# The place of six exponentials in ScalarE's queue: pairs 41 to 43 take the odd slot, pairs 44 to 46 the even one

## The chip, the cores and the metric

The kernel runs on one core of a Trainium2 chip. The metric is the device time in microseconds (us) of one execution; lower is better. The engines are TensorE (PE in the profile, its weight loads PEld), VectorE (DVE), ScalarE (ACT), GpSimd (POOL) and SyncE (SP, which only issues DMAs here). Each works through a queue of its own in the order in which the program wrote it, and waits on semaphores for the others.

## The reference

All in float32. First, attention for 4 batches of 8 heads, 576 tokens, head dimension 64: scores = q kᵀ / 8; of each row of scores only the 32 largest are kept, softmax over them, times v. Then two MLP blocks over the 4 x 576 tokens of width 512. The first mixes x by a real part of a two-dimensional Fourier transform, u = x + Re(FFT2(x)), normalises u over the width, and adds relu(un w1) w2 (512 to 2048 to 512). The second does the same without the transform and with a gain vector. The mask of the 32 largest is what VectorE spends its time on.

```python
kth = np.partition(scores, -top_k, axis=-1)[..., -top_k:-top_k + 1]
scores = np.where(scores >= kth, scores, -1000000000.0)
attn = np.exp(scores - np.max(scores, axis=-1, keepdims=True))
attn = attn / (np.sum(attn, axis=-1, keepdims=True) + 1e-09)
```

## The kernel before

**Tiles, pairs and slots.** The attention is cut into 144 tiles of 128 rows by 576 scores, 36 to a batch, two tiles to a pair (72 pairs). TensorE and ScalarE work in slots, one for each tile: slot s transposes the masked probabilities of tile s (`probs_T`, L684) and copies them out of PSUM (`probs_out`, L927). Each slot also carries pieces of the other work: one or two units of an MLP (`mlp1`, L735: 512 to 128 hidden columns; `mlp2`, L752: back to 512), in odd slots the product with v (`values`, L706 or L700) and its copies, and in slots 76 to 80 the ten pieces of the Fourier transform of batch 1 (`dft_piece`, L779 to L796; copied out by `piece_out`, L958). Which unit lies in which slot is a fixed plan; slots 82 and 87 hold two units. Before a group of units starts, its tokens are turned (`un_T`, L811 on TensorE in slots 86, 87 and 88; `un_out`, L976 and L980 on ScalarE).

**VectorE goes by pairs.** `pair(n)` finds the 32 largest of tiles 2n and 2n+1 in four rounds of MAX8 (L1140), with three rounds of MATCH_REPLACE8 (L1146) between them, and then masks: it multiplies the exponentials `ex` by (score >= 32nd largest) (L1153). The mask waits for the exponentials (`s_exp`); the transposes of slot s wait for the mask of tile s (`s_masked`). After pairs 40, 41 and 42 VectorE also combines the transform's pieces of batch 1 (`combined`, L1217 to L1236), and after pairs 61, 62 and 63 those of batch 2.

**Exponentials.** ScalarE writes `ex` for both tiles of a pair (`exps`, L920, behind a small scaling of the maxima, L915, that waits for the first round of MAX8 of both tiles). In most of the kernel it does so in the even slot s for the pair s/2 + 1, right behind `probs_out(s)`. Where `late_exps(s)` holds, it does so in the odd slot behind it, right behind `probs_out(s + 1)`:

```python
if s % 2 == 0 and s + 2 < TILES and s not in (...) and not late_exps(s):
    exps(s + 2)
    exps(s + 3)
if s % 2 == 1 and late_exps(s - 1):
    exps(s + 1)
    exps(s + 2)
```

Behind them in the same slot of ScalarE's queue come the two copies of the hidden unit (`relu_out`, L989 and L990), which TensorE's next unit and GpSimd's subtraction (L512) wait for, then `un_out`, `piece_out`, the copies of the product with v (L943, L951, L938), and the conversions of the weights for coming units (L1009, L1004). NT is 36. `late_exps` holds before the change for s // 2 in 43, 44, 45 and in 61, 62, 63, that is, for the exponentials of pairs 44, 45, 46 and of pairs 62, 63, 64.

**Scores.** From pair 36 on the scores come back from HBM, where they were set aside; ScalarE issues the load of pair s/2 + 2 in even slots (`scores_in`, L909).

Of the kernel before, what the change touches and what calls it, by code (L numbers as in the profile page):

```python
# [14 lines left out]
NT = NHP * TPP  # L15
# [102 lines left out]

def late_exps(s):

    return s // 2 in (NT + 7, NT + 8, NT + 9, 3 * NT // 2 + 7, 3 * NT // 2 + 8, 3 * NT // 2 + 9)


def scaled_by_act(p):
# [93 lines left out]
def build(nc, q, k, v, g2, w_raw, seq_t, wid_t, alt_t, w_low, sc_ahead, out):  # L218
# [4 lines left out]
    with ctx:  # L223
# [651 lines left out]
        def _(act):  # L875
# [163 lines left out]
            for s in range(SLOTS):  # L1039
                pieces = [(b, i) for b in range(B) for i in range(PIECES) if piece_slot(b, i) == s]  # L1040
                if s < TILES:
                    probs_out(s)
                    if s == START[0]:
                        for t in turns_at(s):
                            un_out(t)
                    if 0 <= s - 2 < AHEAD:
                        scores_aside(s - 2)
                    if s + RING < KEPT:
                        if s not in SCORED.values():
                            scores_out(s + RING)  # L1050
                    elif s % 2 == 0 and s + RING < TILES:
                        scores_in((s + RING) // 2)
                    if s % 2 == 0 and s < 2 * KF:
                        weights_high(s + 1)
                    if 0 <= s - 2 < AHEAD:
                        store_aside(s - 2)
                    if s % 2 == 0 and s + 2 < TILES and s not in (START[0] - 3, START[0] - 1, START[0] + 1) and not late_exps(s):
# [5 lines that stand above are left out]
# [324 lines left out]
```

## Time and profile before

| | |
|---|---|
| Time, median of 3 runs (lowest, highest) | 1359.7 us (1359.5, 1363.7) |
| The profiled execution's own time | 1362.1 us |
| Its span | 1360.3 us |
| Busy share of the span: PE, PEld, DVE, ACT, POOL | 92%, 75%, 81%, 59%, 26% |
| The chain that ended last: PE, DVE, all others | 57%, 36%, 7% |
| Mean granted clock of TensorE | 0.977 of full speed |

The profile is that of one execution. The span runs from the first to the last instruction; the time around it is 1.8 us. A busy share is a mean over stages with different limits. The chain is the work that ended last, followed back from the last instruction, at each step to what released it or to the instruction before it on its engine.

### The profile page before, as it was taken

How to read it: one execution, taken by the hardware profiler on the slowest of the kernel's cores; microseconds unless marked ns; L12 is line 12 of the kernel's file. 1: busy time of each engine (PE TensorE's matmuls, PEld its weight loads, DVE VectorE, ACT ScalarE, POOL GpSimd, SP SyncE). 2: the span in 40 equal slices, each digit the busy share in tenths (PEclk: the TensorE clock that was granted, in tenths of full speed). 3: DMA queues.
4: the chain of work that ended last, by engine and by line, in shares of the span. 5: the costliest groups of instructions: out<-in, count | busy, mean ns of one | idle time of the engine just before them, and what ended most of it. 6: DMA issues, size and time to landing. Idle time of an engine off the chain costs nothing.

```text
span 1360.3 us, 22775 instructions
## 1 busy us (share of the span) xinstructions
PE 1252.0 (92%) x7944; PEld 1024.3 (75%) x7944; DVE 1101.4 (81%) x2196; ACT 798.4 (59%) x1586; POOL 356.6 (26%) x327
## 2 busy tenths in 40 slices
PE   5776778999999899999988999999989999999999
PEld 3444444787777778788876888887679999999997
DVE  7999999899999989999999779975484454646453
ACT  4777765578777646776665557664353434343442
POOL 2444430122232431223335123333030111212110
PEclk9989978999999899999999999999999999999999
DMA  7899993567757757777885577753244343333342
GB/s 249 321 338 340 327 325 145 186 223 252 244 194 259 236 189 251 267 259 241 263 285 197 168 231 238 259 195 129 80 153 142 123 148 117 128 115 127 119 148 85
DMA packets 118259, 282.21 MB, mean 207 GB/s; under 512 B 29825, under 2 KB 29826, under 8 KB 118146
## 3 DMA queue, kind: packets, MB, share of 16 engines
q1 hardware_dynamic: 106386, 233.55, 51.7%
q10 hardware_dynamic: 10368, 42.47, 8.3%
q0 software_dynamic: 1392, 4.73, 1.1%
q8 instruction: 65, 1.06, 0.3%
q14 instruction: 48, 0.39, 0.1%
HBM read 237.44 MB, written 42.73 MB: 206 GB/s over the span
## 4 chain that ended last, share of the span: by engine, by line
PE 57%; DVE 36%; issue 5%; ACT 1%; POOL 1%; DMA 1%; SPq 0%; ACTq 0%; DVEq 0%
PE Big L752 23%; DVE top L1140 15%; PE Big L735 15%; DVE wk L1146 14%; PE Sp L735 7%; DVE ex L1153 3%; PE Tp L684 3%; PE Sp L779 2%; PE Tp L706 2%; PE Sp L791 1%; DVE st L1232 1%; PE Tp L811 1%; PE Big L779 1%; PE Sp L642 1%; PE Big L791 0%
## 5 line engine op out<-in xcount | busy, mean ns | idle before, releaser
L752 PE MATMUL Big<-wr,hh 128*128 128x512 f32 x1152 | 361.4, 395 | 0.0
L735 PE MATMUL Big<-uh,wr 128*128 128x256 f32 (+1 forms) x1400 | 320.9, 319 | 7.1 <-ACT hh L990 6.8
L1140 DVE MAX8 top<-wk 128x8 f32<-128x576 f32 x432 | 304.3, 745 | 0.0
L735 PEld LDWEIGHTS Big<-uh,wr 128*128 128x128 f32 x1400 | 236.5, 191 | 26.3 <-issue 16.5
L752 PEld LDWEIGHTS Big<-wr,hh 128*128 128x128 f32 x1152 | 217.6, 189 | 41.1
L752 PE MATMUL Big<-wr,hl 128*128 128x512 f32 x576 | 238.7, 414 | 4.8 <-DVE wr L1285 4.6
L512 POOL TENSOR_TENSOR hl<-hf,hh 128x256 fp32r<-128x256 f32 (+1 forms) x126 | 108.5, 861 | 452.5 <-ACT hh L990 452.5
L735 PE MATMUL Big<-ul,wr 128*128 128x256 f32 (+1 forms) x700 | 218.6, 312 | 0.0
L1146 DVE MATCH_REPLACE8 wk<-top,wk 128x576 f32<-128x576 f32 x288 | 211.4, 741 | 0.0
L684 PE MATMUL Tp<-ident,ex 128*128 128x128 f32 x720 | 117.1, 289 | 47.2 <-DVE ex L1153 38.3
L927 ACT ACTIVATE pT<-Tp 128x640 f32<-128x640 f32 x144 | 101.1, 702 | 88.1 <-PE Tp L684 87.9
L684 PEld LDWEIGHTS Tp<-ident,ex 128*128 128x128 f32 x720 | 86.5, 146 | 87.6 <-issue 50.8
L990 ACT ACTIVATE hh<-Big 128x384 fp32r<-128x384 f32 (+1 forms) x175 | 75.5, 432 | 118.1 <-PE Big L735 118.1
L1153 DVE SCALAR_TENSOR_TENSOR ex<-sc,top,ex 128x576 f32<-128x576 f32 x144 | 124.6, 902 | 18.8 <-ACT ex L920 18.7
L752 PEld LDWEIGHTS Big<-wr,hl 128*128 128x128 f32 x576 | 108.5, 188 | 34.8 <-issue 15.7
L735 PEld LDWEIGHTS Big<-ul,wr 128*128 128x128 f32 x700 | 133.5, 191 | 0.0
L1140 DVE MAX8 top<-sc 128x8 f32<-128x576 f32 x144 | 101.6, 746 | 16.6 <-ACT sc L886 9.5
L1146 DVE MATCH_REPLACE8 wk<-top,sc 128x576 f32<-128x576 f32 x144 | 105.7, 741 | 0.0
L920 ACT ACTIVATE ex<-sc,nmx 128x576 f32<-128x576 f32 x144 | 104.0, 769 | 2.3
L506 POOL TENSOR_TENSOR wr<-wf,wr 128x1024 fp32r<-128x1024 f32 x32 | 75.3, 2368 | 111.3 <-DVE top L1140 109.3
L989 ACT ACTIVATE hf<-Big 128x256 f32<-128x256 f32 (+1 forms) x126 | 52.2, 414 | 82.0 <-PE Big L735 82.0
L706 PE MATMUL Tp<-pT,vn 128*64 128x128 f32 x1280 | 87.9, 286 | 12.4 <-ACT pT L927 11.9
(136 smaller groups left out, 1832.1 us busy)
## 6 DMA issues: line engine op xcount, KB each, us to landing
wf<-in_weights SPq DMA_DIRECT2D x208, 512.0 KB, 3.6
wr<-w_low SPq DMA_DIRECT2D x252, 256.0 KB, 4.3
sc<-in_weights SPq DMA_DIRECT2D x48, 512.0 KB, 3.2
sc<-sc_ahead ACTq DMA_DIRECT2D x36, 576.0 KB, 5.6
w_low<-wr SPq DMA_DIRECT2D x32, 512.0 KB, 6.6
sc_ahead<-U ACTq DMA_DIRECT2D x18, 576.0 KB, 5.2
sc_ahead<-un ACTq DMA_DIRECT2D x9, 576.0 KB, 4.1
sc_ahead<-yb ACTq DMA_DIRECT2D x9, 576.0 KB, 6.5
```

The costliest lines, as they stand in the source:

```text
L506: pool.tensor_tensor(wr[:, r, :, 1, :], wf[:, j % WFS, :, :], wr[:, r, :, 0, :].bitcast(f32), ALU.subtract).then_inc(s_wlow, 1)
L512: pool.tensor_tensor(hl[:, n % 2, 0:w], hf[:, n % 2, 0:w], hh[:, n % 2, 0:w].bitcast(f32), ALU.subtract).then_inc(s_hl[0], 1)
L684: last = nc.tensor.transpose(Tp[:, c * P:(c + 1) * P], ex[:, s % RING, c * P:(c + 1) * P], ident[:, :])
L706: last = nc.tensor.matmul(OT[h * D:(h + 1) * D, :], vn[:, par, c, h, 0:D], pT[:, h, c * P:(c + 1) * P], start=(c == 0), stop=(c == C - 1))
L735: last = nc.tensor.matmul(hidden(n), a[:, kd * P:(kd + 1) * P], x[:, kd, 0:P * SIZE[p]], start=(kd == 0 and j == 0), stop=(kd == KD - 1 an ...
L752: last = nc.tensor.matmul(Ac[:, j, :], a[:, n % 2, j * P:(j + 1) * P], w, start=(f == 0 and m == 0), stop=(f == KF - 1 and m == 2))
L920: nc.scalar.activation(ex[:, s % RING, 0:S], sc[:, s % RING, :], ACT.Exp, bias=nmx[:, s % RING:s % RING + 1], scale=1.0 / np.sqrt(D)).then ...
L927: nc.scalar.activation(pT[:, s % 2, :], Tp[:, 0:C * P], ACT.Copy).then_inc(s_pT_sb, 1)
L990: nc.scalar.activation(hh[:, n % 2, 0:w], hidden(n), ACT.Relu).then_inc(s_h_sb, 1)
L1140: nc.vector.max(top[:, s % RING, r, :], src).then_inc(s_top, 1)
L1146: nc.vector.match_replace(out=wk[:, a, :], in_to_replace=top[:, s % RING, r, :], in_values=src, imm_value=STRUCK).then_inc(s_struck, 1)
L1153: nc.vector.scalar_tensor_tensor(out=ex[:, s % RING, 0:S], in0=sc[:, s % RING, :], scalar=top[:, s % RING, ROUNDS - 1, 7:8], in1=ex[:, s % ...
```

## The change

One line: the set for which `late_exps` holds. The first three of its six members move from 43, 44, 45 to 40, 41, 42.

```diff
 def late_exps(s):
 
-    return s // 2 in (NT + 7, NT + 8, NT + 9, 3 * NT // 2 + 7, 3 * NT // 2 + 8, 3 * NT // 2 + 9)
+    return s // 2 in (NT + 4, NT + 5, NT + 6, 3 * NT // 2 + 7, 3 * NT // 2 + 8, 3 * NT // 2 + 9)
```

So the exponentials of pairs 41, 42, 43 go from slots 80, 82, 84 to slots 81, 83, 85, and those of pairs 44, 45, 46 from slots 87, 89, 91 to slots 86, 88, 90. No instruction is added or taken away on any engine.

## Rows read from the trace of the kernel before

**Rows 1.** Page, part 1: busy us, share of the span, instructions of each engine.

```profile
PE 1252.0 (92%) x7944; PEld 1024.3 (75%) x7944; DVE 1101.4 (81%) x2196; ACT 798.4 (59%) x1586; POOL 356.6 (26%) x327
```

**Rows 2.** Three stretches: us, then busy by engine (instructions), PEclk, DMA share, GB/s.

```profile
509.00:523.00 14.00, 13.90 (x124) 11.90 (x123) 13.71 (x29) 8.24 (x20) 1.46 (x2) 1.00 0.57 187
...
523.00:552.00 29.00, 26.39 (x199) 22.38 (x197) 28.80 (x65) 18.87 (x43) 6.42 (x10) 0.94 0.76 267
...
699.90:703.30 3.40, 3.36 (x18) 3.16 (x20) 3.40 (x9) 1.95 (x5) 3.06 (x6) 0.50 0.56 187
```

**Rows 3.** The chain that ended last: start, length, what.

```profile
509.23 0.43 DVE xf L1217
...
585.88 0.74 PE Tp L684 x5
...
662.88 0.77 PE Tp L684 x5
```

**Rows 4.** ScalarE in order of time, slots 80 to 87: start, us, instruction, [idle before].

```profile
517.04 0.70 ACT L927 ACTIVATE pT<-Tp 128x640 f32<-128x640 f32 x1 [0.42 <-PE Tp L684]
...
524.10 0.71 ACT L927 ACTIVATE pT<-Tp 128x640 f32<-128x640 f32 x1 [0.31 <-PE Tp L684]
...
542.94 0.20 ACT L915 ACTIVATE nmx<-top 128x2 f32<-128x2 f32 x1 [2.13 <-DVE top L1140]
...
557.55 0.72 ACT L927 ACTIVATE pT<-Tp 128x640 f32<-128x640 f32 x1
```

**Rows 5.** VectorE in order of time.

```profile
522.41 0.80 DVE L1153 SCALAR_TENSOR_TENSOR ex<-sc,top,ex 128x576 f32<-128x576 f32 x1
...
523.87 0.42 DVE L1217 TENSOR_TENSOR xf<-xs 128x257 f32<-128x257 f32 x1
...
537.04 0.80 DVE L1153 SCALAR_TENSOR_TENSOR ex<-sc,top,ex 128x576 f32<-128x576 f32 x1
...
537.76 1.29 DVE L1153 SCALAR_TENSOR_TENSOR ex<-sc,top,ex 128x576 f32<-128x576 f32 x1
...
552.62 1.42 DVE L1140 MAX8 top<-sc 128x8 f32<-128x576 f32 x2
...
774.65 1.26 DVE L1217 TENSOR_TENSOR xf<-xs 128x257 f32<-128x257 f32 x1
...
796.15 0.82 DVE L1153 SCALAR_TENSOR_TENSOR ex<-sc,top,ex 128x576 f32<-128x576 f32 x1 [7.40 <-ACT ex L920]
```

**Rows 6.** ScalarE in order of time, later in the kernel.

```profile
722.11 0.21 ACT L915 ACTIVATE nmx<-top 128x2 f32<-128x2 f32 x1 [1.49 <-DVE top L1140]
...
794.51 0.70 ACT L927 ACTIVATE pT<-Tp 128x640 f32<-128x640 f32 x1 [0.72 <-PE Tp L684]
```

**Rows 7.** TensorE in order of time.

```profile
539.15 0.92 PE L684 MATMUL Tp<-ident,ex 128*128 128x128 f32 x5
...
545.30 0.48 PE L735 MATMUL Big<-uh,wr 128*128 128x256 f32 x2 [1.87 <-ACT hh L990]
...
552.11 0.74 PE L684 MATMUL Tp<-ident,ex 128*128 128x128 f32 x5 [0.54 <-DVE ex L1153]
...
556.00 0.77 PE L684 MATMUL Tp<-ident,ex 128*128 128x128 f32 x5
...
574.62 0.74 PE L684 MATMUL Tp<-ident,ex 128*128 128x128 f32 x5 [0.69 <-DVE ex L1153]
...
585.88 0.74 PE L684 MATMUL Tp<-ident,ex 128*128 128x128 f32 x5 [0.71 <-DVE ex L1153]
...
699.94 0.76 PE L735 MATMUL Big<-uh,wr 128*128 128x256 f32 x2 [3.68 <-ACT hh L990]
...
725.35 0.77 PE L684 MATMUL Tp<-ident,ex 128*128 128x128 f32 x5 [2.21 <-ACT uf L980]
```

**Rows 8.** GpSimd in order of time.

```profile
537.14 1.30 POOL L512 TENSOR_TENSOR hl<-hf,hh 128x256 fp32r<-128x256 f32 x1 [2.62 <-ACT hh L990]
...
774.63 1.00 POOL L512 TENSOR_TENSOR hl<-hf,hh 128x384 fp32r<-128x384 f32 x1 [8.07 <-ACT hh L990]
```

## The prediction

> **What bounds the kernel now.** I read the page's busy shares first. TensorE has the highest, 92% against VectorE's 81% [rows 1], but that is a mean, so I asked for the chain that ended last around the slots that the diff names. The combination that follows pair 40 starts at 509.23, which ties slots and pairs to times: pair 41 is masked from 522.41, pair 42 from 537.04 [rows 5], and ScalarE's copies of slots 80, 81 and 87 start at 517.04, 524.10 and 557.55 [rows 4]. From 509.23 to 585.88 every step of the chain is VectorE's, and from 585.88 to 662.88 nearly every step is TensorE's [rows 3]. In 523 to 552 VectorE is busy for 28.80 of 29.00 us and TensorE for 26.39 [rows 2]. TensorE meets VectorE's masks in slots 86, 90 and 92, where it waits 0.54, 0.69 and 0.71 us for them [rows 7]. So in slots 80 to 92 a microsecond that VectorE loses is lost, and one that ScalarE or TensorE loses is free up to a slack of 0.7 + 0.7 = 1.4 us between slots 87 and 92.
>
> **The change, part by part.**
>
> *Pair 41, from slot 80 to slot 81.* Its exponentials lay behind the copy at 517.04 and were done long before the mask at 522.41. They will lie behind the copy at 524.10, after the mask wants them. Does slot 81 come earlier for it? The copy at 524.10 waits for TensorE, which is busy for 13.90 of the 14.00 us from 509 to 523 [rows 2, 4], on work that waits for nothing of ScalarE's; I take no gain. What a mask needs after a copy when it waits for the exponentials is shown where pair 62 is late already: copy at 794.51, mask at 796.15, 1.64 us [rows 5, 6]. So pair 41's mask starts at 524.10 + 1.64 = 525.74 instead of 522.41: **+3.33 us** on VectorE, in the stretch where it is the chain. Nothing on VectorE lies between to fill it: pair 42's rounds stand behind the mask in its queue.
>
> *Pairs 42 and 43, from slots 82 and 84 to 83 and 85.* Their masks move to 537.04 + 3.3 = 540.3 and some 554.5. Pair 42's exponentials will start near 535, pair 43's near 546 to 548 in slot 85. Both are ready in time: 0, covered by VectorE's own rounds of MAX8, which run for some ten us ahead of each mask. ScalarE's wait of 2.13 us for the maxima of pair 43 (at 542.94) and TensorE's 1.87 us behind it (at 545.30) go [rows 4, 7]. I cost this at nothing, for TensorE only reaches the mask of slot 86 earlier and waits there. If VectorE were not the limit it would be worth 2 us and more (rival below). In slot 84 TensorE, which came to its transposes at 539.15 [rows 7], now has to wait for the mask at 540.3 + 0.8, some 2 us, and in slot 86 it waits for what the delay, its old wait and the 1.87 us that go leave over after those 2 us: 3.3 + 0.5 + 1.9 - 2.0, some 3.7 us or more.
>
> *Collisions of VectorE with GpSimd.* The second mask of pair 42 took 1.29 us instead of 0.80, while GpSimd's subtraction ran from 537.14 for 1.30 [rows 5, 8]. Its mask comes 3.3 us later, when that subtraction is over: **-0.5**. In return the first combination behind pair 41 now falls on a subtraction. When exponentials lie in the odd slot, mask, copies of the unit and subtraction follow in a fixed rhythm: for pair 61 the subtraction starts at 774.63, the combination at 774.65, and takes 1.26 us where the one at 523.87 took 0.42 [rows 5, 8]. The unit is smaller in slot 81 (256 columns against the 384 of [rows 8], so some 0.7 us against 1.00), so I take **+0.5**, between 0 and 0.85.
>
> *Pairs 44 to 46, from slots 87, 89, 91 to 86, 88, 90.* VectorE has these exponentials in time either way: 0 on it. What they move is ScalarE's queue. In slot 86 they come ahead of the copies of the unit and of the turned tokens, which TensorE's transposes of slot 87 wait for. They must wait for the first maxima of pair 44, ready at 552.62 + 1.42 = 554.04 [rows 5] (all times here 3.3 us later in the new trace). The same order is in the trace once: scaling at 722.11, transposes at 725.35 behind a wait of 2.21 us, so 3.24 us from one to the other [rows 6, 7]. Here that gives 554.07 + 3.24 = 557.3 against 556.00 [rows 7]: TensorE 1.3 us late in slot 87. In slot 87 ScalarE is then free of the exponentials and catches up, but TensorE, which works without a pause, does not; slot 88 repeats the order without adding to it. On top comes the clock: after a wait of 3.68 us TensorE's clock was granted at 0.50, its lower level of 1.2 GHz, for 3.40 us [rows 2, 7]. The wait of 3.7 us or more ahead of slot 86 is like it. Half speed over slot 86 hides partly behind ScalarE's exponentials; I take 0.5 us more. Lateness 1.8 against a slack of 1.4: **+0.4**, with bounds of 0 (no fall of the clock) and about 2 (two falls in a row, 1.7 us each, less what hides).
>
> *Sum.* 3.3 - 0.5 + 0.5 + 0.4 = +3.7 us. From 585.88 the chain is TensorE's [rows 3], and each step that follows is released by the one before it, so the delay passes to the end. Against the profiled execution: span 1360.3 to 1364.0, its time 1362.1 to 1365.8. That execution lies 2.4 us above the median of the runs, so the median goes from 1359.7 to **1363.4 us**, +0.27%. About 0.3% (4.1 us) is what a measurement of this kernel can tell from no change, so this is a small loss just under that mark.
>
> **A rule that speaks against this.** The row says that in 523 to 552 VectorE is the fuller engine, 28.80 us against 26.39 [rows 2], though over the whole kernel it is TensorE [rows 1]. The Trainium skill, in Perfetto Trace Analysis, Identifying the Most-Contended Engine, says to optimise the engine with the highest occupancy first. Taken over the whole kernel that is TensorE, and the change would be a gain, as in the second rival. The same page adds that the limit can change from one regime to another, and this trace agrees, by the chain's 76 us on VectorE. Its price by the rule is that rival's, and by the rows it is the sum above.
>
> **Rivals.**
>
> *A. ScalarE's new order in slots 86 to 90 becomes the limit.* If the exponentials of pairs 44 and 45 each hold TensorE as long as at 725.35 (2.21) and the clock falls there (1.7 more), TensorE is 2.2 + 1.3 + 1.7 - 1.4 = 3.8 us behind VectorE in slot 92: 3.3 + 3.8 = +7.1, 1366.8 us. It decides from a lateness of 1.4 us on. For it: my own estimate already is at 1.8. Against it: the second pair's order starts from a late TensorE, so its wait should be gone.
>
> *B. Faster: TensorE is the limit.* The waits of 1.87 us at 545.30 and the half clock behind them (about 1.5 us) go, and VectorE catches up its 3.3: -3.4, 1356.3 us. It needs VectorE to have 3.3 us of idle time between 525 and 586; the row shows 0.2 us in the first 29, and the chain runs through it without a stop. Against it then.
>
> *C. Nothing.* Slot 81 starts earlier since slot 80 has no exponentials, or the exponentials get ahead some other way, so that VectorE does not stall: 1359.7 +/- 1. Against it: TensorE is busy through slot 80 [rows 2], and the copy at 524.10 waited 0.31 us for it [rows 4].
>
> **How the numbers follow.** The forecast's mechanism has 0.80. Its own range: 3.3 without either collision, less 0.9 for collisions that go, is +2.4; 3.3 + 0.85 + 2 is +6.2; so 1362.1 to 1365.9. Of it 0.33 lies above 4.1 us. A has 0.06, B 0.05, C 0.09. Slower by over 0.3%: 0.33 + 0.06 = 0.39; within: 0.47 + 0.09 = 0.56; faster: 0.05. For 8 in 10 I take the likeliest case's range, lowered toward C and raised toward A: 1359.6 to 1366.6.
>
> **What would show it.** In the changed profile: VectorE idle some 3.3 us ahead of pair 41's mask, released by ScalarE's exponentials, mask 1.64 us behind the copy of slot 81; the combination behind it at 1.2 to 0.8 us instead of 0.42; no idle of VectorE ahead of pairs 42 to 46; TensorE waiting about 2 us in slot 84 and about 4 us in slot 86, with the granted clock at 0.50 near there; ScalarE's 2.13 us wait for maxima gone, and one of about half a microsecond in slot 86; TensorE waiting for the turned tokens' copy ahead of slot 87; its transposes of slot 92 at 585.88 + 3.3 to 4. The prediction is wrong if pair 41's mask starts by 523, if the chain between 509 and 586 runs over TensorE, or if slot 92 starts more than 5 us later.

## The result, and the profile after

The changed kernel takes 1364.99 us (median of 10 runs, 1363.41 to 1367.96) against 1360.59 us of the kernel before (10 runs on the same chip, 1358.7 to 1363.7). The ratio is 1.0035, 95% interval [1.0024, 1.0046]: slower by 0.35%, or some 4.8 us by the ratio (4.4 by the medians). The forecast was +3.7 us in a range of -0.1 to +6.9.

The profiled execution of the changed kernel has a span of 1361.6 us, only 1.3 above that of before. To see where the 4 us are one needs a marker that both traces have in the same place. ScalarE's copy of a finished group of MLP units (L998) is one. Its rows in the kernel before, ScalarE in order of time (start, us, instruction, [idle before]):

```profile
488.34 1.02 ACT L998 ACTIVATE yb<-Big 128x1024 f32<-128x1024 f32 x1
...
579.31 1.03 ACT L998 ACTIVATE yb<-Big 128x1024 f32<-128x1024 f32 x1
...
941.28 1.46 ACT L998 ACTIVATE yb<-Big 128x1536 f32<-128x1536 f32 x1 [1.33 <-PE Big L752]
...
1017.43 1.03 ACT L998 ACTIVATE yb<-Big 128x1024 f32<-128x1024 f32 x1 [0.37 <-PE Big L752]
```

And in the changed kernel:

```profile
487.02 1.02 ACT L998 ACTIVATE yb<-Big 128x1024 f32<-128x1024 f32 x1
...
582.26 1.03 ACT L998 ACTIVATE yb<-Big 128x1024 f32<-128x1024 f32 x1
...
944.24 1.46 ACT L998 ACTIVATE yb<-Big 128x1536 f32<-128x1536 f32 x1 [1.34 <-PE Big L752]
...
1018.73 1.03 ACT L998 ACTIVATE yb<-Big 128x1024 f32<-128x1024 f32 x1 [0.37 <-PE Big L752]
```

The stage that holds slots 77 to 90 took 90.97 us before and 95.24 after, +4.27. It is a steady measure: in the four kernels of the experiments that leave these slots as they were before it took 90.93 to 90.96 us. The four stages behind it, to 941, differ by 0.05 us or less each. The stage from there to 1017 took 76.15 and 74.49, -1.66, though nothing in it was changed; the last section says what that is. The time up to the first marker was 1.3 us shorter, though nothing ahead of it was changed either. So one pair of profiled executions shows +1.3, the touched stage alone +4.3, and the medians +4.4.

VectorE of the changed kernel in order of time, to be held against [rows 5]:

```profile
507.90 0.43 DVE L1217 TENSOR_TENSOR xf<-xs 128x257 f32<-128x257 f32 x1 [2.68 <-ACT xs L958]
...
524.41 0.82 DVE L1153 SCALAR_TENSOR_TENSOR ex<-sc,top,ex 128x576 f32<-128x576 f32 x1 [3.25 <-ACT ex L920]
...
525.90 0.96 DVE L1217 TENSOR_TENSOR xf<-xs 128x257 f32<-128x257 f32 x1
...
540.33 0.81 DVE L1153 SCALAR_TENSOR_TENSOR ex<-sc,top,ex 128x576 f32<-128x576 f32 x1
...
564.35 1.21 DVE L1153 SCALAR_TENSOR_TENSOR ex<-sc,top,ex 128x576 f32<-128x576 f32 x1
...
587.01 1.66 DVE L1153 SCALAR_TENSOR_TENSOR ex<-sc,top,ex 128x576 f32<-128x576 f32 x1
```

The first row is the combination behind pair 40, at 509.23 in [rows 3]: the anchor, 1.33 us earlier here. The second is pair 41's mask, with 3.25 us of idle time ahead of it, ended by the exponentials. The mask stands 16.51 us behind the anchor, against 13.18 before: +3.33. The third is the combination that collides, 0.96 against 0.42. The fourth is pair 42's second mask, 0.81 against 1.29. The fifth and sixth are the first masks of pairs 44 and 46, which took 1.07 and 0.94 us before. The last of them in the kernel before:

```profile
584.79 0.94 DVE L1153 SCALAR_TENSOR_TENSOR ex<-sc,top,ex 128x576 f32<-128x576 f32 x1
```

ScalarE of the changed kernel, to be held against [rows 4]:

```profile
515.71 0.70 ACT L927 ACTIVATE pT<-Tp 128x640 f32<-128x640 f32 x1 [0.42 <-PE Tp L684]
...
522.77 0.70 ACT L927 ACTIVATE pT<-Tp 128x640 f32<-128x640 f32 x1 [0.32 <-PE Tp L684]
523.37 0.20 ACT L915 ACTIVATE nmx<-top 128x2 f32<-128x2 f32 x1
523.60 1.44 ACT L920 ACTIVATE ex<-sc,nmx 128x576 f32<-128x576 f32 x2
...
556.15 0.21 ACT L915 ACTIVATE nmx<-top 128x2 f32<-128x2 f32 x1 [0.48 <-DVE top L1140]
```

ScalarE's copies of slots 80 and 81 stand 7.06 us apart, as before, so slot 81 did not come earlier. From its copy at 522.77 to the mask at 524.41 it is 1.64 us, the number read at pair 62.

TensorE, to be held against [rows 7], and two windows on its clock (columns as in [rows 2]):

```profile
540.56 0.74 PE L684 MATMUL Tp<-ident,ex 128*128 128x128 f32 x5 [2.82 <-DVE ex L1153]
...
554.19 0.74 PE L684 MATMUL Tp<-ident,ex 128*128 128x128 f32 x5 [3.61 <-DVE ex L1153]
...
559.59 0.71 PE L684 MATMUL Tp<-ident,ex 128*128 128x128 f32 x5
...
577.27 0.92 PE L684 MATMUL Tp<-ident,ex 128*128 128x128 f32 x5
...
588.83 0.73 PE L684 MATMUL Tp<-ident,ex 128*128 128x128 f32 x5 [0.72 <-DVE ex L1153]
```

```profile
541.50:544.90 3.40, 3.40 (x15) 3.11 (x14) 3.30 (x8) 1.82 (x5) 0.55 (x1) 0.51 0.57 188
555.10:558.50 3.40, 3.40 (x17) 3.30 (x16) 3.40 (x8) 2.89 (x7) 0.06 (x1) 0.51 0.49 173
```

TensorE waits 2.82 and 3.61 us for VectorE in slots 84 and 86, and behind each wait its clock is granted at half, the level of 1.2 GHz. Slot 87 comes 5.40 us behind slot 86 instead of 3.89, so TensorE is 1.5 us late there. It works through all of that time: the row at 559.59 has no wait for the turned tokens' copy ahead of it, which the forecast had named as a sign. In slot 90 (577.27) it no longer waits for VectorE, and in slot 92 it waits 0.72 us, as much as before. Slot 92 stands 80.93 us behind the anchor instead of 76.65: +4.28.

### The profile page after: what moved, and what is told of

It is laid out like the page before. It is cut to its first block, busy times and chain, and to the rows that moved or that the text cites. A ratio compares the mean times of both kernels' runs of the same rounds, so it can differ in the third digit from the quotient of the medians.

```text
span 1361.6 us, 22775 instructions
## 1 busy us (share of the span) xinstructions
PE 1251.4 (92%) x7944; PEld 1025.3 (75%) x7944; DVE 1102.6 (81%) x2196; ACT 799.5 (59%) x1586; POOL 355.8 (26%) x327
## 4 chain that ended last, share of the span: by engine, by line
PE 57%; DVE 34%; issue 5%; POOL 2%; ACT 1%; DMA 1%; SPq 0%; ACTq 0%; DVEq 0%; POOLq 0%
PE Big L752 23%; PE Big L735 15%; DVE top L1140 14%; DVE wk L1146 13%; PE Sp L735 7%; DVE ex L1153 3%; PE Tp L684 2%; PE Sp L779 2%; PE Tp L706 2%; PE Sp L791 1%; PE Tp L811 1%; DVE st L1232 1%; PE Big L779 1%; PE Tp L700 0%; PE Big L791 0%
## 5 line engine op out<-in xcount | busy, mean ns | idle before, releaser
L735 PE MATMUL Sp<-uh,wr 128*128 128x384 f32 (+1 forms) x392 | 96.5, 330 | 0.0
```

Of the source, the lines that this page charges most:

```text
L735: last = nc.tensor.matmul(hidden(n), a[:, kd * P:(kd + 1) * P], x[:, kd, 0:P * SIZE[p]], start=(kd == 0 and j == 0), stop=(kd == KD - 1 an ...
```

## The experiments

All times are ratios or medians against runs of the kernel before on the same chip. The first line of a diff is from the changed kernel where it has NT + 4, NT + 5, NT + 6, and otherwise from the kernel before, if the text does not say it. "Stage" is the time between the first two marker rows above, in the one profiled execution of each kernel: 90.97 us before, 95.24 changed. A stage is read from one trace each, the ratio from 5 to 12 runs of the kernel.

**Pair 41 alone to the odd slot.** Slots 82 to 92 keep the old order.

```diff
-    return s // 2 in (NT + 7, NT + 8, NT + 9, ...)
+    return s // 2 in (NT + 4, NT + 7, NT + 8, NT + 9, ...)
```

> The kernel before with pair 41's exponentials alone moved to the odd slot 81; pairs 44 to 46 keep their odd slots. Theory (VectorE is the limit in slots 80 to 92 and stalls for pair 41): the whole 3.3 us of idle time ahead of pair 41's mask, the combination behind it 0.5 us longer, the slow mask of pair 42 0.5 us shorter, so +3.3 us, 2.5 to 4.3. Rival (the loss is ScalarE's new order in slots 86 to 90, which makes TensorE late): that order is the old one here, so 0 +/- 0.5 us.

Measured: ratio 1.0028 [1.0019, 1.0037], 1363.68 against 1360.53 us; stage 94.35, +3.38. VectorE:

```profile
524.15 0.82 DVE L1153 SCALAR_TENSOR_TENSOR ex<-sc,top,ex 128x576 f32<-128x576 f32 x1 [3.26 <-ACT ex L920]
...
525.63 0.96 DVE L1217 TENSOR_TENSOR xf<-xs 128x257 f32<-128x257 f32 x1
...
540.06 0.81 DVE L1153 SCALAR_TENSOR_TENSOR ex<-sc,top,ex 128x576 f32<-128x576 f32 x1
...
586.60 0.94 DVE L1153 SCALAR_TENSOR_TENSOR ex<-sc,top,ex 128x576 f32<-128x576 f32 x1
```

The stall, the collision that comes and the one that goes are all there, and four fifths of the loss with them (0.28% of 0.35%, 3.38 of 4.27 us). The rival, that ScalarE's order in slots 86 to 90 is the loss, falls.

**Pairs 44 to 46 alone to even slots.**

```diff
-    return s // 2 in (NT + 7, NT + 8, NT + 9, ...)
+    return s // 2 in (...)
```

> The kernel before with the exponentials of pairs 44 to 46 alone moved to the even slots 86, 88, 90; pairs 41 to 43 keep their even slots. Theory: TensorE comes 1.3 to 1.8 us late to slot 88, waits less for VectorE in slots 90 and 92, and the end does not move beyond a collision or two of VectorE with GpSimd: 0 to +1 us, and no idle time of VectorE ahead of pairs 41 to 46. Rival (ScalarE's order in slots 86 to 90 is the loss): the whole loss of the change, +3.5 to +5 us.

Measured: 1.0001 [0.9992, 1.0009]; stage 91.76, +0.79. Pair 44's mask took 1.21 us and pair 46's 1.63, and TensorE waited 1.21 us for the turned tokens in slot 87, but only 0.69 for VectorE in slot 92, as before. The two halves add up: 3.38 + 0.79 = 4.17 against 4.27.

**The change without pair 41.**

```diff
-    return s // 2 in (NT + 7, NT + 8, NT + 9, ...)
+    return s // 2 in (NT + 5, NT + 6, ...)
```

> The changed kernel with pair 41's exponentials back in slot 80; pairs 42 and 43 in the odd slots 83 and 85, pairs 44 to 46 in the even ones. Theory: no stall of VectorE, so 0 to +1 us against the kernel before, and ScalarE's wait for pair 43's maxima (2.13 us) and TensorE's 1.87 us behind it gone without a gain, since TensorE then waits for VectorE's mask in slot 86 for some 1.9 us more. Rival 1 (the loss is in slots 86 to 90): +3.5 us or more. Rival 2 (TensorE limits this stretch, and the change would have gained but for pair 41): -2 to -3.4 us.

Measured: 1.0009 [1.0000, 1.0018], 1360.50 against 1360.53 us; stage 91.92, +0.95. TensorE:

```profile
551.22 1.30 PE L684 MATMUL Tp<-ident,ex 128*128 128x128 f32 x5 [3.90 <-DVE ex L1153]
```

It waits 3.90 us for VectorE in slot 86 and has nothing of it: the 1.87 us that the change frees on TensorE only lengthen its next wait. Rival 2 falls. Behind that wait the clock fell (1.30 us for the five transposes, against 0.74), and slot 87 still begins 5.38 us behind slot 86, only 0.17 later than with pairs 44 to 46 alone (5.21). So the slow stretch hides behind pair 44's exponentials here. That it is not free where they are out of the way, the run with pairs 41 to 45 late shows below.

**Pair 41's exponentials between the two places.** They stand behind the weight conversions of slot 80, with the rest of the change as it is. The diff is against the changed kernel.

```diff
-                    if s % 2 == 1 and late_exps(s - 1):
+                    if s % 2 == 1 and late_exps(s - 1) and s != 2 * (NT + 4) + 1:
...
                     for n in units_at(s):
                         if n not in second_at(s):
                             highs(n)
+                if s == 2 * (NT + 4):
+                    exps(s + 2)
+                    exps(s + 3)
```

> The changed kernel, but pair 41's exponentials stand in ScalarE's queue behind the weight conversions of slot 80, ahead of the last piece's copy, instead of behind the copy of slot 81. By the rows they then start near 522.2 on the old time base and the mask near 523.05 instead of 522.41. Theory (the loss is the time by which the mask waits for the exponentials): a stall of 0.6 us in place of 3.25, so +0.5 to +1.8 us against the kernel before, that is some 2.7 us less than the changed kernel. Rival (what costs is that exponentials were moved at all, or the clock and order in slots 84 to 90): as the changed kernel, +4 to +5 us.

Measured: 1.0016 [1.0005, 1.0026], 1362.30 against 1360.53 us; stage 92.63, +1.66. VectorE (the mask's line is L1156 in this kernel):

```profile
522.37 0.82 DVE L1156 SCALAR_TENSOR_TENSOR ex<-sc,top,ex 128x576 f32<-128x576 f32 x1 [0.54 <-ACT ex L920]
```

The idle time falls by 2.71 us, from 3.25 to 0.54, and the stage by 2.61. So the loss follows the time by which the mask waits, nearly microsecond for microsecond, and not the fact that the exponentials were moved.

**Pair 46 back to the odd slot.** The stretch up to slot 92 held 0.7 us that the forecast had not: pair 46's first mask at 1.66 us.

```diff
-    return s // 2 in (NT + 4, NT + 5, NT + 6, ...)
+    return s // 2 in (NT + 4, NT + 5, NT + 6, NT + 9, ...)
```

> The changed kernel with the exponentials of pair 46 back in the odd slot 91. In the changed kernel pair 46's first mask took 1.66 us and in the kernel before 0.94; GpSimd's subtraction starts at the same moment as the mask (587.02 and 587.01). Theory: this collision is part of the 4.3 us of the stretch, and with pair 46 late the copies of slot 90 come earlier, GpSimd's work on them too, and the mask takes 0.9 to 1.0 us: the stretch from pair 40's combination to slot 92 comes out 0.6 to 0.8 us shorter than in the changed kernel, and the time +3.3 to +4.2 us against the kernel before. Rival (the collision comes from the shift of VectorE by 3.3 us, not from pair 46's slot): the mask stays at 1.6 us.

Measured: 1.0038 [1.0025, 1.0050]; stage 95.26, the same as the changed kernel's. The mask took 1.68 us. The theory that pair 46's slot makes this collision falls, so I took TensorE's lateness behind pairs 44 and 45 for the cause, and tried the reverse.

**Pairs 44 and 45 back to odd slots, pair 46 even.**

```diff
-    return s // 2 in (NT + 4, NT + 5, NT + 6, ...)
+    return s // 2 in (NT + 4, NT + 5, NT + 6, NT + 7, NT + 8, ...)
```

> The exponentials of pairs 41 to 45 in odd slots, pair 46 in the even slot 90 as in the changed kernel. Where pairs 44 to 46 are all even (three kernels) pair 46's first mask took 1.63 to 1.66 us, with pair 46 late alone 1.68, with all three late 0.94. Theory: the collision comes from TensorE's lateness of some 1.5 us behind pairs 44 and 45 in even slots, which moves unit 64 and with it GpSimd's work onto pair 46's mask; with 44 and 45 late it is gone: the mask takes 0.8 to 1.0 us, the stage from the first to the second group's copy after 480 us (pair 40's neighbourhood to slot 90) comes out 3.4 +/- 0.2 us longer than before instead of 4.3, and the time 0.5 to 1 us below the changed kernel's. Rival (it takes only that pair 46 or any one of them is even): the mask stays at 1.6 us.

Measured: 1.0037 [1.0025, 1.0050]; stage 95.78, +4.81. This theory falls too. VectorE, GpSimd and TensorE of this kernel:

```profile
565.19 1.86 DVE L1153 SCALAR_TENSOR_TENSOR ex<-sc,top,ex 128x576 f32<-128x576 f32 x1
...
587.74 1.57 DVE L1153 SCALAR_TENSOR_TENSOR ex<-sc,top,ex 128x576 f32<-128x576 f32 x1
```

```profile
582.06 1.02 POOL L512 TENSOR_TENSOR hl<-hf,hh 128x384 fp32r<-128x384 f32 x1 [5.82 <-ACT hh L990]
584.02 2.51 POOL L528 TENSOR_TENSOR U<-U,yb 128x512 f32<-128x512 f32 x2 [0.94 <-ACT yb L998]
586.83 0.81 POOL L531 DMA_DIRECT2D out<-U  x1 [0.30 <-POOL U L528]
587.66 1.02 POOL L512 TENSOR_TENSOR hl<-hf,hh 128x384 fp32r<-128x384 f32 x1
```

```profile
554.32 0.73 PE L684 MATMUL Tp<-ident,ex 128*128 128x128 f32 x5 [3.62 <-DVE ex L1153]
...
559.71 0.71 PE L684 MATMUL Tp<-ident,ex 128*128 128x128 f32 x5
```

Either is enough. The subtraction at 587.66 ends a queue of GpSimd's work that begins with the subtraction of unit 64 at 582.06. That one comes later against VectorE when TensorE is late (pairs 44 and 45 even), and also when ScalarE writes pair 46's exponentials ahead of unit 64's copies (pair 46 even). With all three in odd slots, as before or with pair 41 alone moved, the subtraction starts 0.72 us ahead of the mask and the mask takes 0.94 us. In the three other cases it starts within 0.1 us of it, and the mask takes 1.57 to 1.68. The larger stage is one more collision: the row at 565.19 is pair 44's second mask, 1.86 us against 0.81 before. That the subtraction is what holds the masks is read from these traces; no run moved the subtraction by itself.

This run also prices the half clock alone. Slot 86 has no exponentials ahead of its copies here, as before, but TensorE's wait of 3.62 us and the half clock behind it are there (granted 0.55 in the 3.4 us from 555.10, all of which TensorE is busy). Slot 87 comes 5.39 us behind slot 86 instead of 3.89, 1.50 late.

**Three runs on where the same rule gives something back.** The kernel before has two exponentials placed against it. Pair 58's stand in an even slot ahead of the copies that TensorE waits 2.21 us for (at 725.35 in [rows 7]), though their mask has time. Pair 62's stand in an odd slot, and VectorE is idle 7.40 us for them [rows 5].

```diff
-    return s // 2 in (NT + 7, NT + 8, NT + 9, 3 * NT // 2 + 7, ...)
+    return s // 2 in (NT + 7, NT + 8, NT + 9, 3 * NT // 2 + 3, 3 * NT // 2 + 7, ...)
```

> The kernel before with one more late pair: the exponentials of pair 58 go from the even slot 114 to the odd slot 115. In the trace of before ScalarE waits 1.49 us there for the maxima of pair 58 (at 722.11), the copies of the turned tokens stand behind the exponentials, TensorE waits 2.21 us for them at 725.35, and the chain goes from them over GpSimd's subtraction and gain (725.38 to 729.27) to TensorE's turning at 729.31 (1.77 us of waiting). The mask of pair 58 is wanted 8 us later (730.32) and slot 115's copy stands at 726.92, so by the 1.64 us from copy to mask it costs VectorE nothing. Theory (an exponential is free in the odd slot as long as copy + 1.64 lies ahead of the mask, and in the even slot it costs what stands behind its wait): -1.5 to -2.5 us. Rival (odd slots are bad for exponentials where VectorE is the limit): +1 us or more.

Measured: 1.0000 [0.9989, 1.0012]. In the trace the stage that holds slot 115 went from 93.64 to 92.31 us, -1.33, and the stage behind 941 us took 77.69 instead of 76.15. The mechanism shows, the gain in the end doesn't. The interval reaches from -1.5 to +1.6 us, so it has the -1.5 us that I expected at least only at its edge, and neither shows nor excludes the stage's -1.33. In the kernels that leave the stage with slot 115 alone it took 93.3 to 94.6 us, so of the -1.33 some 1.0 us is clear of chance.

```diff
-    return s // 2 in (..., 3 * NT // 2 + 7, 3 * NT // 2 + 8, 3 * NT // 2 + 9)
+    return s // 2 in (..., 3 * NT // 2 + 8, 3 * NT // 2 + 9)
```

> The kernel before with the exponentials of pair 62 back in the even slot 122. There VectorE sits idle 7.40 us ahead of pair 62's mask (796.15) and the chain runs from there over VectorE to TensorE's wait at 812.62 (1.14 us). Theory: the mask comes some 5 us earlier, VectorE is no longer on the chain there, and TensorE's wait goes: -0.5 to -1.2 us, less what the copies of the hidden units lose behind the exponentials in slot 122, which has one unit. Rival: TensorE limits this stretch by itself and the exponentials now delay the unit's copies by 1.65 us: 0 to +1.5 us.

Measured: 1.0012 [1.0004, 1.0021], so slower by 1.6 us, against the -0.5 to -1.2 that the theory gave. In the trace the stage that holds slots 122 and on went from 95.96 to 94.89 us, -1.07 as expected there, and the stage behind 941 us took 77.72.

The two together, in two runs of one and the same kernel. The text recorded ahead of the first describes its kernel wrongly: it is not the one with pair 58 late written out again, it also has pair 62 in the even slot. Its expectation of -1.5 to -2.5 us belongs to the other kernel.

```diff
-    return s // 2 in (NT + 7, NT + 8, NT + 9, 3 * NT // 2 + 7, 3 * NT // 2 + 8, 3 * NT // 2 + 9)
+    return s // 2 in (NT + 7, NT + 8, NT + 9, 3 * NT // 2 + 3, 3 * NT // 2 + 8, 3 * NT // 2 + 9)
```

> Pair 58 late (slot 115), all six late pairs of the kernel before kept. It is the same set as the run with pair 58 alone, written out again by another name, and so a measure of how well two builds of one kernel agree: the same time within 0.1%, that is -1.5 to -2.5 us against the kernel before if the theory of the run with pair 58 holds.

Measured: 0.9990 [0.9981, 0.9998], 1359.11 against 1359.63 us.

> Pair 58 late (odd slot 115) and pair 62 even (slot 122), the rest as in the kernel before; the kernel of the run e7, whose text described it wrongly. Stage by stage the traces of e4, e6 and e7 gave -1.3 to -1.6 us for pair 58 and -1.1 us for pair 62, so -2.5 us in the stages that they touch. The stage behind 941 us takes 74.5, 76.2 or 77.7 us with the same instructions, by how long TensorE's clock is at its lower level there, in any kernel; if that is chance, the median comes out -1.0 to -2.7 us against the kernel before; if these kernels meet the longer stretch more often, -0.5 us or less.

Measured: 0.9985 [0.9976, 0.9994], 1358.15 against 1359.63 us; the two stages 92.09 and 94.87 us, -1.55 and -1.09, the stage behind 941 us 76.07. So a version that beats both kernels exists, by 0.10 to 0.15% against the one before, which is small but clear of 1 in both runs. TensorE no longer waits for the turned tokens' copy as at 725.35 in [rows 7], nor for VectorE's mask in the later stage (1.14 us at 812.62 before).

## Why the prediction was right, step by step

*VectorE limits slots 80 to 92.* Right up to slot 86, and shown by two runs: TensorE's freed time is worth nothing (the change without pair 41), and VectorE's idle time is worth its full length (the run with the place in between). Behind slot 86 of the changed kernel it is TensorE that is late, and the paragraphs on pairs 44 to 46 below say how that reaches slot 92.

*Pair 41: +3.33.* Right to the hundredth, 16.51 - 13.18 against the anchor. From copy to mask it is 1.64 us in each of the four kernels that have pair 41 behind the copy of slot 81. It was possible because the trace of before held the same order at pair 62, and because TensorE's full slots 80 and 81 left no way for slot 81 to move.

*Pairs 42 and 43: 0, and TensorE's waits of about 2 and 3.7 us.* No idle time of VectorE ahead of their masks, and waits of 2.82 and 3.61 us, the first 0.8 more than forecast.

*Collisions of -0.5 and +0.5.* Right: 1.29 to 0.81, 0.42 to 0.96. One reading behind the second is off, without harm: pair 61's exponentials stand in an even slot, 120, and not in an odd one. What its row shares with pair 41 is that VectorE waits for them (1.96 us ahead of the mask at 773.16). Pair 62, which is in an odd slot, has the same: subtraction at 797.62, combination at 797.63, 1.28 us.

*Pairs 44 to 46: +0.4 from TensorE's lateness.* This is the mis-sized term of the sum: it measured about +0.9. Both of its parts, a lateness of 1.8 us and a slack of 1.4, were wrong.

The lateness was added up from 1.3 for the exponentials and 0.5 for the clock. Pairs 44 to 46 alone make slot 87 1.32 us late (5.21 instead of 3.89), the half clock alone 1.50 (5.39, pairs 41 to 45 late), and the changed kernel with both 1.51 (5.40). The two hide each other almost wholly.

The slack was taken as 0.7 in slot 90 and 0.7 in slot 92. The first was there: slot 90 no longer waits. The second was not, though slot 92 waits as long as before (0.72 us), for the mask that it waits for is late itself. Pair 46's first mask ends behind a subtraction of GpSimd's, which starts 5.6 us behind that of unit 64, and that one waits for ScalarE's copies of slot 90. GpSimd in the changed kernel, and in the kernel before:

```profile
581.41 1.02 POOL L512 TENSOR_TENSOR hl<-hf,hh 128x384 fp32r<-128x384 f32 x1 [5.42 <-ACT hh L990]
...
587.02 1.02 POOL L512 TENSOR_TENSOR hl<-hf,hh 128x384 fp32r<-128x384 f32 x1
```

```profile
578.46 1.01 POOL L512 TENSOR_TENSOR hl<-hf,hh 128x384 fp32r<-128x384 f32 x1 [5.17 <-ACT hh L990]
...
584.07 1.03 POOL L512 TENSOR_TENSOR hl<-hf,hh 128x384 fp32r<-128x384 f32 x1
```

So what TensorE is late by in slot 90 comes back to it in slot 92 by way of ScalarE, GpSimd and VectorE. In all twelve traces slot 92 starts 6.54 to 6.58 us behind the second marker; that is why the stage, which ends 5 us ahead of the mask, shows +4.27 and slot 92 +4.28. TensorE's account of the term: 1.26 us longer from slot 86 to slot 90, less the wait of 0.69 that goes, and 0.29 more in slot 90, together +0.86. VectorE's account of the same loss is two longer masks, +0.14 at pair 44 and +0.72 at pair 46: 3.33 + 0.54 - 0.48 + 0.14 + 0.72 = 4.25. I had asked of the new order only what it does to TensorE, and not when GpSimd's work would fall.

The recorded rule of the fullest engine was held against TensorE's 92%, the busy share of its matmuls. Its weight loads were busy for 75%, less than VectorE's 81% [rows 1], so the shares alone did not say which engine was the fuller one.

The forecast was called a loss just under the mark of 0.3%; it came out just over. The rivals: A's wait for the turned tokens' copy ahead of slot 87 came with pairs 44 to 46 alone (1.21 us) and not in the changed kernel, where slot 92 stands 4.28 us later and not 7.1; B and C are out by the runs above.

## What to carry to other kernels

Where two engines take turns as the limit, ask of each moved instruction when its own reader wants it, not whether it stands near the work it seems to belong to: here the combinations delay the maxima of pair 41, and that seems to call for later exponentials, but pair 41's mask was 3.3 us too early for slot 81. A place elsewhere in the same trace with the same order of instructions (pair 62, copy to mask 1.64 us) gave the price of the move to 0.01 us. When a shift has been priced, go once more along the engine that is the limit and ask of each of its instructions that can be blocked which GpSimd instruction will now run beside it. And before a wait is counted as slack, ask what the awaited instruction itself hangs on: in slot 92 it hung on the engine whose slack it was to be.

## What the runs showed of the hardware

**The end of a blocked mask.** Pair 46's first mask takes two inputs from SBUF. It ended 0.62 or 0.63 us behind the end of GpSimd's subtraction in all twelve traces: 585.10 and 585.73 before, 588.04 and 588.67 in the changed kernel, 588.68 and 589.31 with pairs 41 to 45 late.

So 0.3 us of overlap cost 0.14 and a full 1.0 us cost 0.86, against a mask of 0.80. It goes the other way too. Before the change the subtraction that starts 0.10 us behind pair 42's first mask (537.14 and 537.04) took 1.30 us [rows 8], where others of its size took 0.74, while that mask took its usual 0.80; the second mask, 0.62 us behind the subtraction's start, then took 1.29. The Trainium skill, in SBUF — State Buffer, Who interferes with whom, says that a VectorE instruction with two inputs in SBUF and a GpSimd instruction that reads SBUF exclude each other, the later one being blocked outright. These rows agree with it. Which one came later they don't always tell: in the changed kernel the mask's record starts at 587.01 and the subtraction's at 587.02, and the mask is the one that took longer.

**A clock that differs between executions of the same instructions.** In the tail, TensorE waits 2.5 us for VectorE's folding near 944 to 952, in each kernel where it was read. What its clock did behind that wait differs. The kernel before, from the end of the wait, and the changed one, from 0.4 us behind it (columns as in [rows 2]; the granted clock is the third from the end):

```profile
948.90:952.30 3.40, 3.38 (x6) 1.58 (x6) 2.43 (x5) 0.00 (x0) 0.00 (x0) 0.52 0.42 139
```

```profile
952.30:955.70 3.40, 3.40 (x14) 2.10 (x13) 1.98 (x4) 0.44 (x1) 0.00 (x0) 1.00 0.43 160
```

And the kernel with pair 58 late, two stretches in a row, from 0.4 us behind the wait:

```profile
947.10:950.50 3.40, 3.40 (x7) 1.47 (x6) 1.99 (x4) 0.40 (x1) 0.00 (x0) 0.51 0.48 164
950.50:953.90 3.40, 3.40 (x9) 2.44 (x8) 0.00 (x0) 0.03 (x1) 0.00 (x0) 0.50 0.42 145
```

The stage behind 941 us took 74.5 us in six of the eleven profiled executions of other kernels (full clock), 76.1 in one and in the kernel before (one stretch at half), and 77.7 in four (two stretches). That is up to 3.2 us in the whole time, three quarters of what the change itself costs. The executions of one kernel spread by 4 to 5 us, and this is one part of that: the two profiles of the kernel with pairs 58 and 62 moved had 77.7 and 76.1; it is also why a profiled span alone could not have judged this change. The three kernels with pair 58 or 62 moved that had 77.7 in their profile came out 1 to 3 us (by the ratio) above what the one or two stages that they change promised. Whether these kernels meet the longer stretch more often or by chance was not settled.
